# Attention scores in 64-row products, one head in each half of the array's rows

## The chip, the cores and the metric

The kernel runs on one core of a Trainium2 chip. A core has TensorE (matmuls; PE in the profile, and PEld for its weight loads), VectorE (DVE), ScalarE (ACT), GpSimd (POOL) and SyncE (SP), which here issues nearly all DMAs. The metric is the time of one execution on the device in microseconds, as the median of several runs.

## What is computed

Attention with 4 batches, 8 heads, 576 positions and 64 dimensions a head, in which each query keeps only its 32 largest scores, and behind it two feed-forward layers (512 to 2048 to 512) over the 2304 rows.

```python
scores = scale * np.matmul(q, k.transpose(0, 1, 3, 2))
kth = np.partition(scores, -32, axis=-1)[..., -32:-31]
scores = np.where(scores >= kth, scores, -1e9)
attn = softmax(scores)                      # over the keys
x = concat_heads(attn @ v)                  # 2304 x 512
h = x @ w_in;   x = g(h) @ w_out            # g: 0 below -1, h above 1, (h + 1)^2 / 4 between
h = np.maximum(x @ w_in2, 0); out = (h * h) @ w_out2
```

## The kernel before

**Precision.** Scores and the feed-forward products need more than one pass of the fast fp32r type. Each operand is split into a part "hi" (rounded to fp32r) and a rest "lo", and hi x hi, hi x lo and lo x hi are summed in PSUM.

**Slots.** Attention runs in 72 slots. A slot takes two units t = 0 and 1, each of 128 queries against all 576 keys. In slots 0 to 63 ("normal") the two units are the two heads of a pair, for the same 128 queries of one batch. In slots 64 to 71 ("packed") a unit holds the last 64 queries of both heads of a pair. Slots 0 to 3 ("raw") use unsplit fp32 inputs straight from kq0, with 64 dimensions on 64 rows of the array: head t lies on rows 64t to 64t + 63 (score_raw, L569, in two matmuls of 288 keys; fp32 makes two instructions of each).

**A slot on the engines.** Order is written out by hand in the slot() of each engine; engines meet only through semaphores.
- TensorE in slot n: scores of unit (n+1, 0), transposes of the probabilities of (n-1, 0) (turn_main, L623), scores of (n+1, 1), transposes of (n-1, 1) (L623, L629), then probabilities times v of slot n-1 (times_v, L645 and L650). Between these stand up to three steps of the feed-forward layers: up (L691, 12 matmuls) and down (L719 for the first layer, L725 for the second, 12 of 256 or 6 of 512 columns), placed by the table UP_POS, from slot 10 on.
- ScalarE copies the scores from PSUM into one of four tiles s_sb (copy_scores, L800), which it may do once the mask of the unit four earlier is done, and computes the exponentials (L821).
- VectorE finds the 32nd largest score with four MAX8 and three MATCH_REPLACE8 passes a unit (rank, L1054 and L1056), fourteen a slot. Its first pass over unit (n, t) waits for that unit's copy.
- POOL compares (L1232) and multiplies the mask in (L1237); turn_main waits for that.
- SP loads and stores. Of each pair of heads, keys and queries come once as kq_lo, are split into kq_hi and kq_lo and stored to kq_scratch (restack, L394, L395), and come back as ks (L399) and qs (L406) for each use.

**The score block before.** Rows of kq are interleaved by head (d, h), so that the reload in the form "(x d) h c" puts the hi part of one head on rows 0 to 63 and its lo part on rows 64 to 127, with the two heads side by side in the columns. One matmul over 128 rows thus gives hi x hi + lo x lo with variant 0 of the queries (hi over lo) and the two mixed products with variant 1 (lo over hi); kq_scratch has a third plane, a second copy of the hi queries, to make variant 1. A normal unit takes four matmuls of 288 keys (L588), a packed one ten (L598, L601, L603, L606), since both heads have to be summed into one tile.

score_ps has two PSUM banks, columns 0 to 287 and 512 to 799; the next unit's scores wait until ScalarE has copied them (s_copied).

## Time and profile before

| | us |
|---|---|
| median of 3 runs | 1234.5 (1234.43 to 1236.56) |
| profiled execution | 1234.88 |
| its span in the trace | 1233.1 |
| TensorE busy (matmuls) | 1178.1 |
| VectorE busy | 839.2 |
| ScalarE busy | 776.8 |
| POOL busy | 740.9 |

The span is what the trace covers; 1.8 us of the execution lie around it. Busy times are sums over the whole span, and the engines' shares change from stretch to stretch: up to about slot 10 there is attention alone, then attention and feed-forward steps together until 915 us, then feed-forward steps alone. The records give a matmul's length from its start to its modelled end, and the next one starts before that end; the distance between two starts is what a matmul costs in a dense row. A few matmul records are missing. "L588" is line 588 of the kernel before.

### The profile page before, as it was taken

What the parts mean: (1) busy time and instruction counts of PE and PEld (TensorE: products, weight loads), DVE (VectorE), ACT (ScalarE), POOL (GpSimd) and SP (SyncE); (2) the same over time, 40 slices, a digit from 0 to 9 for tenths busy, and PEclk for the clock granted to TensorE, in tenths of its full rate; (3) what the DMA queues carried; (4) which work ended last, traced back from release to release, by engine and by line L of the source; (5) the groups of instructions that cost most, each with busy time, mean ns of one, the idle gap of its engine ahead of it and who ended that gap; (6) DMA issues with size and microseconds to landing.
All of it is one profiled execution on the core that took longest, in us unless ns stands there. A gap on an engine that the chain in (4) does not pass through costs nothing.

```text
span 1233.1 us, 23032 instructions
## 1 busy us (share of the span) xinstructions
PE 1178.1 (96%) x8184; PEld 1092.9 (89%) x8184; DVE 839.2 (68%) x1863; ACT 776.8 (63%) x1672; POOL 740.9 (60%) x589
## 2 busy tenths in 40 slices
PE   6777899999999999999999999999999999999998
PEld 4667888998889999999999999999999888998887
DVE  7999999999987799899899987878740111110000
ACT  7877666786765767767776665666654544653343
POOL 6868786888977767777676766665652222222222
PEclk9967999999999999999999999999999999999999
DMA  6767886777869932334458831456339500780000
GB/s 253 278 242 262 283 320 259 267 244 308 331 225 396 383 113 99 136 111 138 138 189 296 299 116 40 141 189 191 126 131 368 194 1 1 313 336 1 1 35 18
DMA packets 94914, 239.45 MB, mean 194 GB/s; under 512 B 7760, under 2 KB 46672, under 8 KB 82512
## 3 DMA queue, kind: packets, MB, share of 16 engines
q1 hardware_dynamic: 94640, 237.71, 53.4%
q8 instruction: 66, 1.08, 0.3%
q14 instruction: 48, 0.39, 0.1%
q10 hardware_dynamic: 160, 0.26, 0.1%
HBM read 166.12 MB, written 71.83 MB: 193 GB/s over the span
## 4 chain that ended last, share of the span: by engine, by line
PE 74%; POOL 9%; ACT 7%; issue 4%; DVE 3%; DMA 2%; SPq 1%; ACTq 0%; POOLq 0%
PE h_ps L691 22%; PE y_ps L725 11%; PE y_ps L719 10%; PE pv_ps L650 6%; PE score_ps L691 6%; PE tr_ps L623 4%; PE score_ps L588 3%; POOL s_sb L1232 3%; POOL prob L1237 3%; POOL kq_lo L1215 2%; PE y_ps L711 2%; PE y_ps L714 2%; PE tr_ps L714 2%; PE tr_ps L711 2%; DVE top L1054 1%
## 5 line engine op out<-in xcount | busy, mean ns | idle before, releaser
L691 PE MATMUL h_ps<-xt_ks,w_in 128*128 128x256 f32 (+1 forms) x2628 | 384.8, 296 | 2.2 <-ACT rg L931 1.4
L691 PEld LDWEIGHTS h_ps<-xt_ks,w_in 128*128 128x128 f32 x2628 | 341.8, 191 | 12.3 <-ACT rg L931 1.9
L1250 POOL TENSOR_TENSOR g_lo<-rg,g_hi 128x256 fp32r<-128x256 f32 x224 | 169.4, 756 | 281.6 <-ACT g_hi L949 165.8
L1054 DVE MAX8 top<-rest 128x8 f32<-128x576 f32 x432 | 304.5, 746 | 0.4
L1232 POOL TENSOR_SCALAR s_sb<-s_sb,top 128x576 f32<-128x576 f32 x126 | 222.1, 1763 | 33.8 <-DVE top L1054 33.8
L1056 DVE MATCH_REPLACE8 rest<-top,rest 128x576 f32<-128x576 f32 x288 | 211.4, 741 | 0.0
L1237 POOL TENSOR_TENSOR prob<-s_sb,prob 128x576 f32<-128x576 f32 x128 | 183.0, 1432 | 14.9 <-ACT s_sb L842 3.1
L719 PE MATMUL y_ps<-g_hi,w_out 128*128 128x256 f32 x896 | 180.9, 285 | 4.9 <-POOL g_lo L1250 4.5
L725 PE MATMUL y_ps<-w_out,g_hi 128*128 128x512 f32 x448 | 158.6, 395 | 0.8 <-ACT moves L910 0.7
L719 PEld LDWEIGHTS y_ps<-g_hi,w_out 128*128 128x128 f32 x896 | 147.6, 192 | 7.0 <-POOL g_lo L1250 5.7
L650 PE MATMUL pv_ps<-v_sb,pt 128*128 128x65 f32 x1024 | 129.9, 283 | 0.0
L650 PEld LDWEIGHTS pv_ps<-v_sb,pt 128*128 128x128 f32 x1024 | 128.1, 204 | 0.0
L719 PE MATMUL y_ps<-g_lo,w_out 128*128 128x256 f32 x448 | 126.8, 283 | 0.0
L800 ACT ACTIVATE s_sb<-score_ps 128x576 f32<-128x576 f32 x143 | 91.9, 643 | 48.7 <-PE score_ps L588 27.2
L623 PE MATMUL tr_ps<-ident,prob 128*128 128x128 f32 x576 | 95.5, 292 | 17.8 <-POOL prob L1237 17.6
L1054 DVE MAX8 top<-s_sb 128x8 f32<-128x576 f32 x144 | 102.3, 743 | 14.9 <-ACT s_sb L800 14.8
L1117 DVE SCALAR_TENSOR_TENSOR rg<-rg 128x256 f32<-128x256 f32 x112 | 62.8, 561 | 63.7 <-ACT rg L942 63.4
L1056 DVE MATCH_REPLACE8 rest<-top,s_sb 128x576 f32<-128x576 f32 x144 | 105.6, 739 | 0.1
L821 ACT ACTIVATE prob<-s_sb,neg_max 128x576 f32<-128x576 f32 x128 | 99.4, 776 | 2.1
L725 PEld LDWEIGHTS y_ps<-w_out,g_hi 128*128 128x128 f32 x448 | 84.6, 189 | 17.4 <-issue 1.2
L588 PE MATMUL score_ps<-xt_ks,qs_g 128*128 128x288 f32 x480 | 91.0, 315 | 7.4 <-DMA qs_g<-kq_scratch 6.2
L623 PEld LDWEIGHTS tr_ps<-ident,prob 128*128 128x128 f32 x576 | 72.2, 149 | 27.1 <-issue 20.1
(122 smaller groups left out, 1819.9 us busy)
## 6 DMA issues: line engine op xcount, KB each, us to landing
w_in<-w_scratch SPq DMA_DIRECT2D x32, 1024.0 KB, 7.1
w_out<-w_scratch SPq DMA_DIRECT2D x32, 1024.0 KB, 8.2
xt_ks<-kq_scratch SPq DMA_DIRECT2D x46, 576.0 KB, 6.4
qs_g<-kq_scratch SPq DMA_DIRECT2D x152, 128.0 KB, 4.2
w_scratch<-w_in SPq DMA_DIRECT2D x16, 1024.0 KB, 7.3
w_scratch<-w_out SPq DMA_DIRECT2D x16, 1024.0 KB, 7.0
v_sb<-in_vv_dram SPq DMA_DIRECT2D x48, 325.0 KB, 6.4
moves<-in_w_dram SPq DMA_DIRECT2D x27, 512.0 KB, 6.5
```

Source lines behind the costliest of these rows:

```text
L588: last = pe.matmul(score_ps[:, 512 * half:512 * half + HALF], qq[:, t, var, :], kk[:, t, HALF * half:HALF * (half + 1)], start=(var == 0), ...
L623: last = pe.transpose(tr_ps[t][:, P * j:P * (j + 1)], prob[n % 2][:, base + P * j:base + P * (j + 1)], ident[:, :])
L650: last = pe.matmul(pv_ps[:, V1 * t:V1 * (t + 1)], pt[:, base + P * j:base + P * (j + 1)], vb[:, V1 * (2 * j + t):V1 * (2 * j + t + 1)], st ...
L691: last = pe.matmul(h_bank(k), wi[:, f // 2, w, m, cols], x_part(k, x, m), start=(m == 0 and n == 0), stop=(m == KT - 1 and n == 2))
L719: last = pe.matmul(y_ps[i][:, CHUNK * (m % 2):CHUNK * (m % 2 + 1)], wo[:, f // 2, w, f % 2, P * m:P * (m + 1)], g[f % 2][:, :], start=(f = ...
L725: last = pe.matmul(y_ps[i][:, :], g[f % 2][:, P * i:P * (i + 1)], wo[:, f // 2, w, f % 2, :], start=(f == 0 and n == 0), stop=(f == FT - 1 ...
L821: act.activation(pr[:, SEQ * t:SEQ * (t + 1)], s_sb[i][:, :], ACT.Exp, bias=bias[:, t:t + 1], scale=SCALE).then_inc(exp_done, 1)
L1054: dve.max(best, src[:, :]).then_inc(rank_step, 1)
L1056: dve.match_replace(rest[t][:, :], best, src[:, :], LOWEST).then_inc(rank_step, 1)
L1232: pool.tensor_scalar(s[:, :], s[:, :], top[n % 2][:, t, TOPK - 1:TOPK], None, ALU.is_ge).then_inc(keep_done, 1)
L1237: pool.tensor_tensor(pr[:, cols], s[:, :], pr[:, cols], ALU.mult).then_inc(masked, 1)
L1250: pool.tensor_tensor(lo_of(k), u_of(k), hi_of(k).bitcast(F32), ALU.subtract).then_inc(g_lo_done, 1)
```

## The change

**Layout.** Rows of kq are now head-major: head h on rows 64h to 64h + 63, hi and lo in two planes x of ks and qs. kq_scratch loses its third plane. A load of qs is one DMA, not two, and the third store of restack is gone. For packed slots a new load_tail_ks brings the keys in three DMAs, so that both heads' keys stand in the same order.

**Normal slots from 4 on.** Unit t no longer stands for head t in the score block, but for half t of the keys. Three products (hi x hi, hi x lo, lo x hi) are made for either head on its own 64 rows of the array, head h into bank h: six matmuls of 64 rows and 288 keys, with the head as inner loop. The copy of block t goes to half t of both heads' tiles, so that VectorE's first pass (rank) waits for both copies of the slot.

**Packed slots.** Six matmuls of 128 rows and 288 keys; the queries of the other head are zeros in the layout.

**Tiles.** Six score tiles in three pairs instead of four, and the copy waits for the masks of the slot three earlier. qs_g is half as large; the corner of the second packed unit moves to kq_lo, and the wide jobs' tiles for odd steps to g_all.

```diff
-    kq_dram = [scratch(f"kq_scratch{g}", [3, 2 * DIM, KQ]) for g in range(PREPS)]
+    kq_dram = [scratch(f"kq_scratch{g}", [2, P, KQ]) for g in range(PREPS)]
...
-        s_sb = [sb(f"s_sb{i}", [P, SEQ]) for i in range(4)]
+        s_pairs = sb("s_pairs", [P, 3, 2 * SEQ])
+        s_sb = [s_pairs[:, i // 2, SEQ * (i % 2):SEQ * (i % 2 + 1)] for i in range(6)]
...
+        def in_halves(n):
+
+            return RAW_SLOTS <= n < NORMAL
...
-                sp.dma_start(kq_dram[g][2, :, SEQ:KQ], kq_hi[:, SEQ:KQ].bitcast(F32)).then_inc(restacked, 16)
...
                 sp.dma_start(ks[i][:, :, :].bitcast(F32),
-                             kq_dram[g][0:2, :, 0:SEQ].rearrange("x (d h) c -> (x d) h c", h=2)
+                             kq_dram[g][:, :, 0:SEQ].rearrange("x p c -> p x c")
                              ).then_inc(ks_loaded[i], 16)
+
+            def load_tail_ks(g, i):
+                sp.wait_ge(restacked, 16 * 2 * (PREP_ORDER.index(g) + 1))
+                for rows, to, cols in ((slice(0, DIM), slice(0, SEQ), slice(0, SEQ)),
+                                       (slice(DIM, P), slice(0, MAIN), slice(TAIL, SEQ)),
+                                       (slice(DIM, P), slice(MAIN, SEQ), slice(0, TAIL))):
+                    sp.dma_start(ks[i][rows, :, to].bitcast(F32),
+                                 kq_dram[g][:, rows, cols].rearrange("x p c -> p x c")
+                                 ).then_inc(ks_loaded[i], 16)
 
             def load_qs(g, t, i):
                 cols = slice(SEQ + P * t, SEQ + P * (t + 1))
-                for var in range(2):
-                    sp.dma_start(qs[i][:, :, var, :].bitcast(F32),
-                                 kq_dram[g][var:var + 2, :, cols].rearrange("x (d h) n -> (x d) h n", h=2)
-                                 ).then_inc(qs_loaded[i], 16)
+                sp.dma_start(qs[i][:, :, :].bitcast(F32),
+                             kq_dram[g][:, :, cols].rearrange("x p n -> p x n")).then_inc(qs_loaded[i], 16)
...
-                    for var in range(2):
-                        for half in range(2):
-                            last = pe.matmul(score_ps[:, 512 * half:512 * half + HALF], qq[:, t, var, :],
-                                             kk[:, t, HALF * half:HALF * (half + 1)],
-                                             start=(var == 0), stop=(var == 1))
+                    for i, (x, y) in enumerate(products):
+                        for h in range(2):
+                            rows = slice(DIM * h, DIM * (h + 1))
+                            last = pe.matmul(score_ps[:, 512 * h:512 * h + HALF], qq[rows, x, :],
+                                             kk[rows, y, HALF * t:HALF * (t + 1)],
+                                             start=(i == 0), stop=(i == 2))
...
-                    for var in range(2):
+                    for i, (x, y) in enumerate(products):
                         for half in range(2):
-                            pe.matmul(score_ps[:, 512 * half:512 * half + HALF], qq[:, 0, var, :],
-                                      kk[:, 0, HALF * half:HALF * (half + 1)],
-                                      start=(var == 0), stop=False, skip_group_check=True)
...
+                            last = pe.matmul(score_ps[:, 512 * half:512 * half + HALF], qq[:, x, :],
+                                             kk[:, y, HALF * half:HALF * (half + 1)],
+                                             start=(i == 0), stop=(i == 2))
...
-                if u >= 4:
-                    act.wait_ge(masked, u - 3)
+                if n >= 3:
+                    act.wait_ge(masked, 2 * (n - 3) + 2)
...
+                if in_halves(n):
+                    pair = s_pairs[:, n % 3, :].rearrange("p (h k) -> p h k", h=2)
+                    act.activation(pair[:, :, HALF * t:HALF * (t + 1)], banks, ACT.Copy).then_inc(s_copied, 1)
+                    return
...
                 if op == 0:
-                    dve.wait_ge(s_copied, 2 * n + t + 1)
+                    dve.wait_ge(s_copied, 2 * n + (2 if in_halves(n) else t + 1))
...
-            rows, tail_rows = slice(hh, P, 2), slice(DIM * hh, DIM * (hh + 1))
+            rows = tail_rows = slice(DIM * hh, DIM * (hh + 1))
```

Below stands the built order of instructions at the places of which the prediction speaks. Rows read: line, operation, what it writes <- what it reads, size, how many in a row.

TensorE, a normal slot with first-layer steps, before: y_ps<-g_hi is the last down matmul, score_ps the score block, tr_ps the transposes, h_ps the next up step.

```order
L719 MATMUL y_ps<-g_lo,w_out 128x256
L719 MATMUL y_ps<-g_hi,w_out 128x256
L588 MATMUL score_ps<-xt_ks,qs_g 128x288 x4
L623 MATMUL tr_ps<-ident,prob 128x128 x4
L629 MATMUL tr_ps<-ident,prob 128x128
L691 MATMUL h_ps<-xt_ks,w_in 128x256 x12
```

The same place in the changed program:

```order
L737 MATMUL y_ps<-g_all,w_out 128x256 x12
L614 MATMUL score_ps<-xt_ks,qs_g 128x288 x6
L641 MATMUL tr_ps<-ident,prob 128x128 x4
L647 MATMUL tr_ps<-ident,prob 128x128
L709 MATMUL h_ps<-xt_ks,w_in 128x256 x12
```

The block stands where it stood, between down and the transposes, with six matmuls for four (the rows don't print that each reads 64 rows). The down steps are the same twelve; they read as one row since g_hi and g_lo are now one tensor.

TensorE, a packed slot with second-layer steps, before:

```order
L725 MATMUL y_ps<-w_out,g_hi 128x512
L598 MATMUL score_ps<-xt_ks,qs_g 128x288 x2
L601 MATMUL score_ps<-xt_ks,qs_g 128x288
L603 MATMUL score_ps<-xt_ks,qs_g 128x224
L606 MATMUL score_ps<-xt_ks,qs_g 128x64
L598 MATMUL score_ps<-xt_ks,qs_g 128x288 x2
L601 MATMUL score_ps<-xt_ks,qs_g 128x288
L603 MATMUL score_ps<-xt_ks,qs_g 128x224
L606 MATMUL score_ps<-xt_ks,qs_g 128x64
L623 MATMUL tr_ps<-ident,prob 128x128 x4
```

and in the changed program:

```order
L743 MATMUL y_ps<-w_out,g_all 128x512 x6
L624 MATMUL score_ps<-xt_ks,qs_g 128x288 x6
L641 MATMUL tr_ps<-ident,prob 128x128 x4
L709 MATMUL h_ps<-xt_ks,w_in 128x256 x12
L743 MATMUL y_ps<-w_out,g_all 128x512 x6
```

Ten matmuls with small ones among them have become six equal ones, at the same place.

## Rows read from the trace of the kernel before

**Rows 1.** The page, part 1: busy us (share of the span) xinstructions.

```profile
PE 1178.1 (96%) x8184; PEld 1092.9 (89%) x8184; DVE 839.2 (68%) x1863; ACT 776.8 (63%) x1672; POOL 740.9 (60%) x589
```

**Rows 2.** Busy time in stretches (from:to us), length, engines, granted clock, DMA share, GB/s.

```profile
core 0: us, PE busy (x) PEld busy (x) DVE busy (x) ACT busy (x) POOL busy (x), PEclk, DMA share, GB/s
40.00:200.00 160.00, 130.95 (x881) 121.45 (x881) 156.83 (x354) 116.80 (x225) 123.92 (x78) 0.87 0.76 277
200.00:788.00 588.00, 579.52 (x4567) 560.55 (x4565) 528.64 (x1166) 405.25 (x919) 434.15 (x334) 1.00 0.59 211
788.00:915.00 127.00, 126.74 (x924) 119.15 (x923) 94.02 (x228) 77.79 (x189) 80.62 (x79) 1.00 0.48 154
74.00:77.00 3.00, 2.92 (x12) 2.10 (x10) 3.00 (x9) 2.64 (x5) 3.00 (x3) 0.50 0.96 362
```

**Rows 3.** Score matmuls of normal blocks, 200 to 788 us: count, ns min/median/max, first and last.

```profile
L588 PE MATMUL score_ps<-xt_ks,qs_g x360: 291/295/401, 205.0 to 775.2; 128*128 128x288 f32 x180
```

**Rows 4.** Timeline, PE, a block at full clock: start us, length us (a row's whole), instruction.

```profile
570.13 0.28 PE L719 MATMUL y_ps<-g_hi,w_out 128*128 128x256 f32 x1
570.25 0.69 PE L588 MATMUL score_ps<-xt_ks,qs_g 128*128 128x288 f32 x4
570.78 0.60 PE L623 MATMUL tr_ps<-ident,prob 128*128 128x128 f32 x4
571.14 0.36 PE L691 MATMUL h_ps<-xt_ks,w_in 128*128 128x256 f32 x1
```

**Rows 5.** Timeline, PE, raw scores of slots 0 and 1.

```profile
4.66 0.85 PE L569 MATMUL y_ps<-pt 64*128 64x288 f32 x1
5.01 0.69 PE L569 MATMUL score_ps<-pt 64*128 64x288 f32 x1
5.30 0.68 PE L569 MATMUL y_ps<-pt 64*128 64x288 f32 x1
5.49 0.68 PE L569 MATMUL score_ps<-pt 64*128 64x288 f32 x1
...
7.75 2.29 PE L569 MATMUL score_ps<-pt 64*128 64x288 f32 x4 [0.80 <-ACT s_sb L796]
```

**Rows 6.** Timeline, PE, edges of blocks: into 64 rows, out, and without change of rows.

```profile
22.02 0.42 PE L623 MATMUL tr_ps<-ident,prob 128*128 128x128 f32 x1
22.37 0.84 PE L569 MATMUL score_ps<-rg 64*128 64x288 f32 x1
...
23.97 0.69 PE L569 MATMUL score_ps<-rg 64*128 64x288 f32 x1
24.58 0.69 PE L623 MATMUL tr_ps<-ident,prob 128*128 128x128 f32 x2
...
75.47 0.44 PE L588 MATMUL score_ps<-xt_ks,qs_g 128*128 128x288 f32 x1
75.71 0.41 PE L623 MATMUL tr_ps<-ident,prob 128*128 128x128 f32 x1
```

**Rows 7.** Timeline, PEld (weight loads), the load behind the transposes.

```profile
571.11 0.19 PEld L691 LDWEIGHTS h_ps<-xt_ks,w_in 128*128 128x128 f32 x1
```

**Rows 8.** Waits of PE from 200 to 790 us, the longest: us in total, times, longest.

```profile
PE tr_ps L623 <- POOL prob L1237: 4.1, 7, 1.1
```

**Rows 9.** Timeline, PE, a packed block: its first matmuls and the transposes behind it.

```profile
826.40 0.42 PE L598 MATMUL score_ps<-xt_ks,qs_g 128*128 128x288 f32 x2
...
827.56 0.66 PE L623 MATMUL tr_ps<-ident,prob 128*128 128x128 f32 x4
```

**Rows 10.** Timeline, DVE and ACT, start of slot 6; in brackets idle time and what ended it.

```profile
66.56 0.74 DVE L1054 MAX8 top<-s_sb 128x8 f32<-128x576 f32 x1
67.82 0.76 DVE L1054 MAX8 top<-s_sb 128x8 f32<-128x576 f32 x1 [0.52 <-ACT s_sb L800]
...
67.15 0.64 ACT L800 ACTIVATE s_sb<-score_ps 128x576 f32<-128x576 f32 x1
```

**Rows 11.** DMA issues: out<-in engine xcount, KB each, us to landing.

```profile
qs_g<-kq_scratch SPq DMA_DIRECT2D x152, 128.0 KB, 4.2
...
kq_scratch<-kq_hi SPq DMA_DIRECT2D x16, 320.0 KB, 4.7
```

More of the change, by code:

```diff
@@ L224, in build @@
         neg_max = [sb(f"neg_max{i}", [P, 2]) for i in range(2)]
-        prob = [sb(f"prob{i}", [P, 2 * (MAIN + P)]) for i in range(2)]
+        prob = [sb(f"prob{i}", [P, 2 * SEQ]) for i in range(2)]
         pt = sb("pt", [P, 2 * (MAIN + P)])
@@ L231, in build @@
         g_sb = [rg[:, 2 + i, :] for i in range(2)]
-        g_hi = [sb(f"g_hi{i}", [P, CHUNK], F32R) for i in range(2)]
-        g_lo = [sb(f"g_lo{i}", [P, CHUNK], F32R) for i in range(2)]
+        g_all = sb("g_all", [P, 4 * CHUNK], F32R)
+        g_hi = [g_all[:, 2 * CHUNK * i:2 * CHUNK * i + CHUNK] for i in range(2)]
+        g_lo = [g_all[:, 2 * CHUNK * i + CHUNK:2 * CHUNK * (i + 1)] for i in range(2)]
         ident = sb("ident", [P, P])
@@ L358, in lo_of, with s_of, corner @@
         def lo_of(k):
-            return (kq_hi, qs_g)[k % 2][:, 2 * CHUNK:4 * CHUNK] if wide(k // FT) else g_lo[k % 2][:, :]
+            if not wide(k // FT):
+                return g_lo[k % 2][:, :]
+            return kq_hi[:, 2 * CHUNK:4 * CHUNK] if k % 2 == 0 else g_all[:, 2 * CHUNK:4 * CHUNK]
+        def s_of(u):
+            return s_sb[u % 6]
+        def corner(n, t):
+            if t == 0:
+                return prob[n % 2][:, MAIN:MAIN + P]
+            return kq_lo[:, P * (n % 2):P * (n % 2 + 1)].bitcast(F32)
+        def in_halves(n):
+            return RAW_SLOTS <= n < NORMAL
         def raw(p):
@@ L579, in score @@
                     return
-                if not packed(n):
-                    if n % 2 == 0:
-                        pe.wait_ge(ks_loaded[(n // 2) % 2], 16 * (n // 4))
+                products = ((0, 0), (0, 1), (1, 0))
+                if in_halves(n):
                     if t == 0:
-                        pe.wait_ge(qs_loaded[n % 2], 16 * 2 * (n // 2 - 1))
+                        if n % 2 == 0:
+                            pe.wait_ge(ks_loaded[(n // 2) % 2], 16 * (n // 4))
+                        pe.wait_ge(qs_loaded[n % 2], 16 * (n // 2 - 1))
@@ L597, in score @@
                         for half in range(2):
-                            pe.matmul(score_ps[:, 512 * half:512 * half + HALF], qq[:, 0, var, :],
-                                      kk[:, 0, HALF * half:HALF * (half + 1)],
-                                      start=(var == 0), stop=False, skip_group_check=True)
-                        pe.matmul(score_ps[:, 0:HALF], qq[:, 1, var, :], kk[:, 1, TAIL:TAIL + HALF],
-                                  start=False, stop=(var == 1), skip_group_check=True)
@@ L603, in score @@
-                        pe.matmul(score_ps[:, 512:512 + MAIN - HALF], qq[:, 1, var, :],
-                                  kk[:, 1, TAIL + HALF:SEQ],
-                                  start=False, stop=(var == 1), skip_group_check=True)
-                        last = pe.matmul(score_ps[:, 512 + MAIN - HALF:512 + HALF], qq[:, 1, var, :],
-                                         kk[:, 1, 0:TAIL],
-                                         start=False, stop=(var == 1), skip_group_check=True)
+                            last = pe.matmul(score_ps[:, 512 * half:512 * half + HALF], qq[:, x, :],
+                                             kk[:, y, HALF * half:HALF * (half + 1)],
+                                             start=(i == 0), stop=(i == 2))
@@ L630, in turn_shared @@
                 if packed(n):
-                    last = pe.transpose(tr_ps[0][:, P:2 * P], prob[n % 2][:, 2 * MAIN + P:2 * MAIN + 2 * P],
+                    last = pe.transpose(tr_ps[0][:, P:2 * P], corner(n, 1),
                                         ident[:, :])
@@ L795, in copy_scores @@
                     for half in range(2):
-                        last = act.activation(s_sb[1][:, HALF * half:HALF * (half + 1)], y_ps[half][:, 0:HALF],
+                        last = act.activation(s_of(1)[:, HALF * half:HALF * (half + 1)], y_ps[half][:, 0:HALF],
                                               ACT.Copy)
@@ L811, in exponentiate @@
             def exponentiate(n, t):
-                i = (2 * n + t) % 4
+                s = s_of(2 * n + t)
                 if t == 0:
@@ L824, in exponentiate @@
                     base = (MAIN + P) * t
-                    act.activation(pr[:, base:base + MAIN], s_sb[i][:, 0:MAIN], ACT.Exp,
+                    act.activation(pr[:, base:base + MAIN], s[:, 0:MAIN], ACT.Exp,
                                    bias=bias[:, t:t + 1], scale=SCALE)
                     for hh in range(2):
-                        rows, col = slice(TAIL * hh, TAIL * (hh + 1)), base + MAIN + TAIL * hh
-                        last = act.activation(pr[rows, col:col + TAIL], s_sb[i][rows, MAIN:SEQ], ACT.Exp,
+                        rows = slice(TAIL * hh, TAIL * (hh + 1))
+                        last = act.activation(corner(n, t)[rows, rows], s[rows, MAIN:SEQ], ACT.Exp,
                                               bias=bias[rows, t:t + 1], scale=SCALE)
@@ L1318, in lay_out @@
             vv[:, p, tail_rows, at + DIM] = 1.0
-    for hh in range(2):
-        kq0[:, DIM * hh:DIM * (hh + 1)] = kq[0, 0:RAW_SLOTS // 2, hh::2, 0:RAW]
+    kq0[:] = kq[0, 0:RAW_SLOTS // 2, :, 0:RAW]
     blocks = []
```

41 lines of the change are left out of this document (21 added, 20 removed).

## The prediction, made before the changed kernel ran

> **What bounds the kernel now.** The page's first part comes first: TensorE is busy 96% of the span, VectorE 68% [rows 1]. Those are averages, so the span is next cut into stretches by what limits them [rows 2]. From 40 to 200 us VectorE is busy 156.8 of 160 us (the 14 rank passes of each slot) and TensorE only 131: here only what delays VectorE costs time, and TensorE has 29 us to spare. From 200 to 788 us TensorE is busy 579.5 of 588 us and VectorE 528.6. "Busy" flatters TensorE, whose ends are modelled, so I checked it by distances between starts: around 570 us matmul follows matmul without a hole, 0.12 us apart at 256 columns and 0.13 at 288 [rows 4], and in the whole stretch TensorE's longest wait in sum is the one of L623 for POOL's mask, 4.1 us [rows 8]. So from 200 us on, whatever is put on TensorE's queue is paid in full. 788 to 915 us (packed slots) is the same, 126.7 of 127. Behind it no scores are made. The granted clock is 1.00 (2.4 GHz) from 200 us on, 0.87 on average before.
>
> So the change is to be counted on TensorE: 90 score blocks lie in the bound stretch (360 recorded matmuls of L588, four to a block [rows 3]), 28 more lie ahead of it, and 16 packed blocks lie behind.
>
> **Part 1, the normal score block: six 64-row matmuls for four 128-row ones.** The block now: last matmul of down() starts at 570.13, the four scores at 570.25, the transposes behind them at 570.78 [rows 4]. That is 0.12 + 0.53 = 0.65 us from the last down matmul to the first transpose, nothing lost at either edge.
>
> Do the two halves of the array work side by side? The trace has one place that tells, the first slot, where the raw scores of both heads stand in the queue together: rows 0 to 63 write score_ps, rows 64 to 127 y_ps. score_ps starts at 5.01 and 5.49, y_ps between them at 5.30 [rows 5] and again at 5.78, so each half steps by 0.48 us. Where one half works alone, four such matmuls take 2.29 us with 0.69 for the last, again about 0.5 a step [rows 5, 6]. The halves do not slow each other. So six matmuls should take three steps of 0.13 us instead of four: **-0.13 us a block**.
>
> What do the edges cost? The same raw blocks stand between 128-row transposes. No granted clock is recorded there, but a transpose is 0.42 long as at 75 us [rows 6], where the granted clock is 0.50, that is 1.2 GHz [rows 2]. The last 64-row matmul starts at 23.97 and is 0.69 long; its own step is 0.48, yet the transpose behind it starts only at 24.58, 0.61 later, about 0.07 before the modelled end of the 64-row one [rows 6]. Two more such edges, at 32.8 and 36.1 us, are 0.61 too. The other way, the transpose from 22.02 is 0.42 long and the 64-row matmul starts at 22.37, again 0.07 before the end, 0.35 after it where the transposes' own step is 0.21 [rows 6]. The counter-example is the 128-row block at 75 us: the last L588 starts at 75.47, is 0.44 long, and the transpose behind it starts at 75.71, 0.24 later [rows 6], the plain step of 288 columns at that clock, with 0.2 of the earlier one still to run. So TensorE empties itself whenever the number of rows changes, and nothing else in these places differs in the same manner: rows decide, not the kind of matmul. The Trainium skill says this as a rule (TensorEngine Tiling (Array Packing), Key Properties: changing the tiling mode drains the engine); it gives no duration, and by that rule the trace agrees.
>
> The drain also takes away that the next weights are loaded ahead. At full clock a weight load that was not ahead starts at 571.11 [rows 7], and the matmul it serves starts at 571.14 but is 0.36 long instead of 0.28 [rows 4]: its stream starts 0.11 after the load.
>
> Worked out at full clock, from those rows (an estimate, since no row shows a change of rows at 2.4 GHz):
> - into the block: 0.28 - 0.07 = 0.21 instead of 0.12, and 0.11 for the load: +0.20 us
> - out of it: 0.30 - 0.07 = 0.23 instead of 0.13, and 0.05 for the transposes' load (at half clock 24.58 + 0.69 - 0.42 = 24.85, so 0.27 to the second one instead of 0.21 [rows 6]): +0.15 us
> - three steps for four: -0.13 us
>
> That is **+0.21 us a block**, and 90 x 0.21 = **+19 us**. Both ends: without any edge cost -0.13 (-12 us); with loads in turn (below) +0.48 (+43 us).
>
> The 28 blocks before 200 us cost TensorE as much or more, some 7 us, in its 29 us of slack: nothing, as long as the copy behind them isn't late for VectorE (part 3).
>
> **Part 2, the packed block: six 128-row matmuls for ten.** Now 826.40 to 827.56, 1.16 us [rows 9]; six of 288 columns are 6 x 0.13 = 0.79. No change of rows here. 16 x 0.37 = **-6 us**, all on the bound engine. The keys come in three DMAs instead of one, issued a slot ahead of their use and behind nothing new, so the two more issues stay hidden.
>
> **Part 3, both heads from one pair of copies.** VectorE's first pass over a unit now waits for the second copy, not for the first. In most slots that copy is 2 to 5 us ahead. In slot 6 it isn't: the first pass starts at 66.56, the second copy runs from 67.15 to 67.79, and the second pass already waits 0.52 [rows 10]. The first pass would start at 67.82 too: 0.74 us more. Slots 4 and 8 are like it, together at most 1.9 us in the stretch that VectorE bounds. In nine or so slots after 365 us the copy is late as well, but there VectorE has slack; at worst some of the 0.74 comes back as TensorE waiting for a mask, 5 us at most. Against it: with three pairs of score tiles the copy waits for a mask one slot older. TensorE's waits for POOL are the 4.1 us of [rows 8], and longer slots give VectorE and POOL more room, so down to -4. I take **+1.5**, near the early slots, which have rows.
>
> **Part 4, DMA and SP.** 76 of 152 loads of qs and the 16 third stores of 320 KB go [rows 11]: 15 MB less, and 92 issues fewer on SP (less 32 more for the packed keys). TensorE waits for none of them after 200 us, so 0; below, -1 from the early slots. The wide jobs' tiles have only moved: 0.
>
> **Sum.** +19 - 6 + 1.5 = +14.5 us on the profiled execution's 1234.9 (span 1233.1 and 1.8 around it), that is 1249.4; the median of the runs lies 0.4 lower: **1249**. Its own range by the bounds is 1242 to 1258.
>
> **Rivals.**
> *The loads of the two halves go in turn.* A load takes the 0.11 of [rows 7], and the rows at the start of the program are too wide apart to show whether two loads run together. If they queue, six loads are 0.66 us and become the step: 0.27 more a block, 90 x 0.48 - 6 + 1.5 = +39, **1274**. For it: loads are the densest thing the engine does. Against it: the halves behaved as independent in all else. The Trainium skill states that a load's time depends on columns, not rows (TensorE: Matmul & The Clock Gate, LDWEIGHTS), so that twelve loads a slot would cost half as much again as eight; it also has loads overlap where row groups differ (Part 3 of the same page). No run here shows which.
>
> *A gain: no drain in the dense stream.* If the edge cost seen at half clock came from an empty queue and is hidden when the queue is full, each block saves its 0.13: -12 - 6 = -18, **1217**. It decides if the edge costs under 0.13 a block. Against it: three edges agree within 0.01 us, and the semaphores of the two later ones had long been reached. The Trainium skill's table of theoretical speed-up (TensorEngine Tiling, Overview), twice for contractions up to 64, gives this sign.
>
> *Half the edge cost.* If the loads do go ahead and only the emptying is paid, 0.09 + 0.09 - 0.13 = 0.05 a block: +4.5 - 6 + 1.5 = 0, **1235**, no change.
>
> *VectorE becomes the bound* through the later first pass: 12 slots at 0.74 on top of the forecast, up to **1258 to 1266**.
>
> **How the numbers follow.** Forecast 0.52, loads in turn 0.18, gain 0.12, half the edge 0.10, VectorE 0.08. The range of 1234 to 1276 holds all but the gain and a part of the half-edge case. A measurement here can tell 0.2%, 2.5 us, from no change: faster 0.13, same 0.08, slower 0.79.
>
> **What would show it.** On the timeline around a normal block after 200 us: about 0.32 us from the last down matmul to the streaming of the first score, pairs of starts 0.13 apart, and 0.28 to the transposes; the mean length of a slot 0.4 us up; 788 to 915 shorter by 6 us; the part behind it unchanged in length. Pairs 0.21 apart mean the loads go in turn. Starts without a hole at the edges mean I was wrong about the drain, and the time falls.

## The result and the profile after

The changed kernel takes **1242.6 us** (median of 5 runs, 1242.14 to 1244.64); the kernel before, on the same chip, 1234.9 (5 runs). The ratio is 1.0062 with a 95% interval of 1.0052 to 1.0073: **0.6% slower**. The forecast was 1249.0 with a range of 1234 to 1276. The sign and the mechanism held, but its sum was 14.5 us and only 8.4 came in the span. The profiled execution of the changed kernel took 1243.26 us, its span is 1241.5, against 1233.1 before. Of one kernel below, m_four_edges, the profiled execution ran at a granted clock of about 0.55 from 118 us on and took 1971 us, so its time is that of its three other runs.

Part 1 of the page and the stretches of [rows 2], now of the changed kernel (busy us, share of the span or number of instructions in brackets; in the second view then the granted clock, the DMA share and GB/s):

```profile
PE 1197.5 (96%) x8360; PEld 1077.0 (87%) x8360; DVE 841.8 (68%) x1863; ACT 777.8 (63%) x1672; POOL 742.8 (60%) x589
...
40.00:200.00 160.00, 142.00 (x950) 125.11 (x950) 157.61 (x357) 117.67 (x226) 124.42 (x79) 0.86 0.71 256
200.00:788.00 588.00, 582.91 (x4655) 537.23 (x4655) 520.08 (x1142) 399.07 (x904) 427.05 (x327) 1.00 0.53 191
788.00:915.00 127.00, 123.85 (x886) 115.80 (x886) 101.74 (x242) 80.48 (x196) 82.67 (x80) 1.00 0.57 141
```

The bound is where it was. From 40 to 200 us TensorE has 11 us more to do and takes them from its slack: VectorE is busy 157.6 of 160 us, 156.8 in [rows 2]. From 200 us on TensorE is busy 583 of 588 us. The number that stands out is in the third stretch: TensorE was busy 126.74 of 127 us there [rows 2] and is now busy 123.85.

A normal block at full clock answers to [rows 4]. Timeline, PE and then PEld, changed kernel (start us, length us, instruction). The view joins neighbours into one row; rows cut narrower are shown between:

```profile
567.31 0.28 PE L737 MATMUL y_ps<-g_all,w_out 128*128 128x256 f32 x1
567.52 0.40 PE L614 MATMUL score_ps<-xt_ks,qs_g 64*128 64x288 f32 x2
567.52 0.53 PE L614 MATMUL score_ps<-xt_ks,qs_g 64*128 64x288 f32 x4
567.52 0.66 PE L614 MATMUL score_ps<-xt_ks,qs_g 64*128 64x288 f32 x6
567.89 0.29 PE L614 MATMUL score_ps<-xt_ks,qs_g 64*128 64x288 f32 x2
568.12 0.66 PE L641 MATMUL tr_ps<-ident,prob 128*128 128x128 f32 x4
...
567.52 0.19 PEld L614 LDWEIGHTS score_ps<-xt_ks,qs_g 64*128 64x128 f32 x2
567.52 0.30 PEld L614 LDWEIGHTS score_ps<-xt_ks,qs_g 64*128 64x128 f32 x4
```

- In: 567.31 to 567.52, 0.21 us instead of 0.12, and the first pair is 0.40 long instead of 0.29, since its load, at 567.52 too, was not ahead.
- Inside: two matmuls start together, and each further pair ends 0.13 later (0.40, 0.53, 0.66). The loads behave alike: two take 0.19, four 0.30. Both halves load and stream side by side (in the records two matmuls of a pair start 3 to 4 ns apart).
- Out: the last pair starts at 567.89, the transposes at 568.12, 0.23 later. Four of them are 0.66 long instead of 0.60, the load again.

Over the 76 blocks between 240 and 780 us with a down step ahead, the median from its last matmul to the first transpose is 0.822 us, against 0.656 before, and the transposes behind take 0.057 more: 0.88 against 0.66, **+0.22 us a block**. The forecast had +0.21.

The score matmuls in the stretch of [rows 3], and TensorE's waits there, against [rows 8] (us in total, times, longest):

```profile
L614 PE MATMUL score_ps<-xt_ks,qs_g x540: 286/292/405, 204.4 to 787.0; 64*128 64x288 f32 x180
...
PE tr_ps L641 <- POOL prob L1259: 3.1, 8, 0.9
```

**Where the 8.4 us are.** The score blocks of slots 4 to 71 stand on TensorE in the same order in both kernels, so each block's start can be compared. They are numbered from 4 (slot 4, unit 0) to 139 (slot 71, unit 1). Differences of the starts, after less before:

| block | before us | after us | difference |
|---|---|---|---|
| 16 | 100.84 | 100.46 | -0.4 |
| 38 | 230.14 | 229.64 | -0.5 |
| 124, the first packed one | 783.54 | 795.49 | +11.9 |
| 139, the last | 888.39 | 897.15 | +8.8 |

So up to 230 us the new blocks cost nothing. Of the 86 distances from block to block behind it, 59 grew by 0.19 to 0.25 us, together 12.9; the other 27 sum to -0.4. In 18 of these 27 a wait of TensorE for POOL, ScalarE or another engine stands in the trace of the kernel before. Two more (43 and 45) grew by 0.5 and 1.1, with new waits of some 0.3 us in the changed kernel, and seven grew by 0.05 to 0.13 with no wait on record in either. What the 18 are shows at one of them. Timeline, PE, before and after, with the wait in brackets:

```profile
595.59 0.69 PE L588 MATMUL score_ps<-xt_ks,qs_g 128*128 128x288 f32 x4
596.65 0.63 PE L623 MATMUL tr_ps<-ident,prob 128*128 128x128 f32 x4 [0.37 <-POOL prob L1237]
```

```profile
602.91 0.68 PE L614 MATMUL score_ps<-xt_ks,qs_g 64*128 64x288 f32 x6
603.76 0.63 PE L641 MATMUL tr_ps<-ident,prob 128*128 128x128 f32 x4 [0.16 <-POOL prob L1259]
```

Block to transposes took 1.06 us before, though a block that waits for nothing takes 0.53 [rows 4]: TensorE stood still for 0.53 us, of which the row shows 0.37, since the matmul ahead has a modelled end. After, the transposes again start when POOL's mask is there, 0.85 us on, and the longer block has only filled the hole.

**The packed slots.** Timeline, PE, changed kernel, the block that answers to [rows 9], and block 134, some 30 us later:

```profile
835.79 0.95 PE L624 MATMUL score_ps<-xt_ks,qs_g 128*128 128x288 f32 x6
836.58 0.60 PE L641 MATMUL tr_ps<-ident,prob 128*128 128x128 f32 x4
...
866.32 1.03 PE L624 MATMUL score_ps<-xt_ks,qs_g 128*128 128x288 f32 x6 [2.30 <-DMA qs_g<-kq_scratch]
```

A block is 0.79 long as forecast, and its transposes are 0.60 long where [rows 9] had 0.66: they no longer stand behind a 64-column matmul. Each distance shrank by 0.43 (from the last block to the end it is 0.38), 16 x 0.43 = -6.9 us. One alone, into block 134 (the scores of slot 69, whose loads SP issues in its slot 67; the expectations call the place slot 67), grew by 2.8: it holds the wait of 2.30, and without it would have shrunk as well, so it costs 3.2. That wait was not there before. Some 0.6 of the other 0.9 are two waits for ScalarE in the same distance, a new one of 0.16 (the h_ps row) and one of 0.69 where before it was 0.26 (the y_ps rows); they stand in the other kernels with six-matmul packed blocks too (a, c, g, i, k and l). Waits of TensorE from 788 to 915 us, changed kernel and then before (us in total, times, longest):

```profile
PE y_ps L743 <- ACT moves L932: 0.7, 1, 0.7
PE h_ps L709 <- ACT rg L953: 0.2, 1, 0.2
...
PE y_ps L725 <- ACT moves L910: 0.3, 1, 0.3
```

SP's queue ahead of it, changed kernel and then kernel before (start us, length us, line, out<-in):

```profile
847.47 0.36 SPq L519 DMA_DIRECT2D moves<-y_scratch  x1
857.79 0.34 SPq L506 DMA_DIRECT2D out_dram<-moves  x1
858.22 1.92 SPq L425 DMA_DIRECT2D xt_ks<-kq_scratch  x3
860.19 0.60 SPq L431 DMA_DIRECT2D qs_g<-kq_scratch  x1
```

```profile
849.24 0.34 SPq L482 DMA_DIRECT2D out_dram<-moves  x1
849.68 0.53 SPq L399 DMA_DIRECT2D xt_ks<-kq_scratch  x1
850.26 1.39 SPq L406 DMA_DIRECT2D qs_g<-kq_scratch  x2
```

In both kernels SP has nothing issued for about 10 us ahead of the store of a finished output tile (from 847.47 to 857.79 here), and the loads of keys and queries stand behind it. Before, the store went 6.2 us ahead of the score block that needs them (855.41), and the loads were just in time. Now three key DMAs of 1.92 us stand ahead of the queries, and the queries take longer to land: 5.8 us in the median of the stretch from 855 to 870, against 4.4 from 848 to 858 in the kernel before. Why is not shown: a store of 512 KB stands ahead of them in both. (DMA issues: KB each, us from issue to landing, changed kernel.)

```profile
out_dram<-moves SPq DMA_DIRECT2D x1, 512.0 KB, 3.6
qs_g<-kq_scratch SPq DMA_DIRECT2D x3, 128.0 KB, 5.8
```

Together: -0.5 + 12.4 - 6.9 + 3.2 = +8.2 us, and +8.4 in the span.

### The profile page after: what moved, and what is told of

Same layout as the page of the kernel before. It is cut to its first block, busy times and chain, and to the rows that moved or that the text cites. A ratio compares the mean times of both kernels' runs of the same rounds, so it can differ in the third digit from the quotient of the medians.

```text
span 1241.5 us, 23292 instructions
## 1 busy us (share of the span) xinstructions
PE 1197.5 (96%) x8360; PEld 1077.0 (87%) x8360; DVE 841.8 (68%) x1863; ACT 777.8 (63%) x1672; POOL 742.8 (60%) x589
## 4 chain that ended last, share of the span: by engine, by line
PE 78%; POOL 7%; DVE 5%; ACT 4%; issue 2%; DMA 2%; SPq 0%; ACTq 0%; POOLq 0%
PE h_ps L709 23%; PE y_ps L743 11%; PE y_ps L737 10%; PE pv_ps L668 7%; PE score_ps L709 6%; PE tr_ps L641 5%; PE score_ps L614 4%; DVE top L1076 3%; POOL s_pairs L1254 2%; DVE rest L1078 2%; POOL prob L1259 2%; PE y_ps L729 2%; PE y_ps L732 2%; PE tr_ps L729 2%; PE tr_ps L732 2%
## 5 line engine op out<-in xcount | busy, mean ns | idle before, releaser
L1272 POOL TENSOR_TENSOR g_all<-rg,g_all 128x256 fp32r<-128x256 f32 x224 | 170.0, 759 | 292.9 <-ACT g_all L971 162.5
L1254 POOL TENSOR_SCALAR s_pairs<-s_pairs,top 128x576 f32<-128x576 f32 x126 | 223.5, 1774 | 31.2 <-DVE top L1076 31.2
L1259 POOL TENSOR_TENSOR prob<-s_pairs,prob 128x576 f32<-128x576 f32 x128 | 182.6, 1429 | 16.0 <-DVE top L1076 4.5
L737 PE MATMUL y_ps<-g_all,w_out 128*128 128x256 f32 x1344 | 180.7, 284 | 3.1 <-POOL g_all L1272 3.1
L743 PE MATMUL y_ps<-w_out,g_all 128*128 128x512 f32 x672 | 174.1, 394 | 0.7 <-ACT moves L932 0.7
L737 PEld LDWEIGHTS y_ps<-g_all,w_out 128*128 128x128 f32 x1344 | 169.1, 191 | 5.2 <-POOL g_all L1272 4.3
L743 PEld LDWEIGHTS y_ps<-w_out,g_all 128*128 128x128 f32 x672 | 119.1, 189 | 21.5 <-issue 0.9
L1076 DVE MAX8 top<-s_pairs 128x8 f32<-128x576 f32 x144 | 101.8, 742 | 19.1 <-ACT s_pairs L823 10.0
L1078 DVE MATCH_REPLACE8 rest<-top,s_pairs 128x576 f32<-128x576 f32 x144 | 105.5, 738 | 0.1
L843 ACT ACTIVATE prob<-s_pairs,neg_max 128x576 f32<-128x576 f32 x128 | 99.2, 775 | 2.1
```

What stands on the lines that cost most here:

```text
L737: last = pe.matmul(y_ps[i][:, CHUNK * (m % 2):CHUNK * (m % 2 + 1)], wo[:, f // 2, w, f % 2, P * m:P * (m + 1)], g[f % 2][:, :], start=(f = ...
L743: last = pe.matmul(y_ps[i][:, :], g[f % 2][:, P * i:P * (i + 1)], wo[:, f // 2, w, f % 2, :], start=(f == 0 and n == 0), stop=(f == FT - 1 ...
L843: act.activation(pr[:, SEQ * t:SEQ * (t + 1)], s[:, :], ACT.Exp, bias=bias[:, t:t + 1], scale=SCALE).then_inc(exp_done, 1)
L1076: dve.max(best, src[:, :]).then_inc(rank_step, 1)
L1078: dve.match_replace(rest[t][:, :], best, src[:, :], LOWEST).then_inc(rank_step, 1)
L1254: pool.tensor_scalar(s[:, :], s[:, :], top[n % 2][:, t, TOPK - 1:TOPK], None, ALU.is_ge).then_inc(keep_done, 1)
```

## The experiments

Twelve kernels ran. Each ratio is against the kernel before as timed beside that kernel. "Block" below is the median from the last matmul ahead to the first transpose, as above.

### What a block is made of: a to d

**a_four128** makes four matmuls of 128 rows in the changed kernel's layout and order.

```diff
-                    for i, (x, y) in enumerate(products):
+                    for i, (x, y) in enumerate(products[0:2]):
                         for h in range(2):
-                            rows = slice(DIM * h, DIM * (h + 1))
+                            rows = slice(0, P)
...
-                                             start=(i == 0), stop=(i == 2))
+                                             start=(i == 0), stop=(i == 1))
```

> The changed kernel, but a normal score block is four 128-row matmuls of 288 keys (two of the three products, over all 128 rows, so the scores of both heads are summed and the lo x hi product is left out). Everything else of the change stays: copies in halves, three pairs of tiles, fewer DMAs, six-matmul packed blocks. If changing the number of rows is what costs: 0.12 us into the block, four steps of 0.13, 0.13 out of it, 0.65 us in all instead of 0.86, the 59 or so blocks that pay give back 0.21 each, about 1230 us, and faster than the kernel before by what the packed blocks bring. If the later first pass of VectorE or the copies are what costs: no less than 1240.

**b_six128** has the line of rows alone changed: all six matmuls on 128 rows.

```diff
-                            rows = slice(DIM * h, DIM * (h + 1))
+                            rows = slice(0, P)
```

> The changed kernel, but each of the six matmuls of a normal block reads all 128 rows (the scores of both heads are summed). No change of rows at the edges, and no two matmuls side by side. Drain theory: 0.12 + 5 x 0.13 + 0.14, 0.91 us a block against 0.86, so 59 x 0.05 = +3 us, about 1246. If the edges cost nothing and the six matmuls themselves are the price: the same 1242 to 1243 with the same block. If two halves side by side were worth nothing: the block would be shorter than in the changed kernel, below 1240.

**c_four64** has the first and the last line of a's diff: four matmuls of 64 rows.

> The changed kernel with four 64-row matmuls a block (the lo x hi product is left out). Drain theory: one step of 0.13 less, both edges unchanged at 0.21 and 0.22: 0.73 us a block, about 59 x 0.13 = 8 us less, 1235. It differs from four 128-row matmuls by the edges less two steps, 0.08 a block. If the price lies in the matmuls (loads in turn): 0.21 less a block or more, 1230 or less.

| | us | ratio, 95% interval | in | block | between transposes | block 38 to 124 |
|---|---|---|---|---|---|---|
| before | 1234.5 | 1 | 0.120 | 0.656 | 0.108 | 0 |
| changed kernel | 1242.6 | 1.0062 (1.0052 to 1.0073) | 0.209 | 0.822 | 0.165 | +12.4 |
| a_four128 | 1229.4 | 0.9958 (0.9944 to 0.9972) | 0.120 | 0.653 | 0.109 | -0.9 |
| b_six128 | 1248.2 | 1.0111 (1.0096 to 1.0126) | 0.120 | 0.918 | 0.108 | +17.7 |
| c_four64 | 1233.1 | 0.9988 (0.9979 to 0.9998) | 0.209 | 0.674 | 0.165 | +4.3 |

Blocks of a, b and c in the timeline (start us, length us):

```profile
572.74 0.69 PE L614 MATMUL score_ps<-xt_ks,qs_g 128*128 128x288 f32 x4
573.26 0.60 PE L641 MATMUL tr_ps<-ident,prob 128*128 128x128 f32 x4
```

```profile
571.45 0.96 PE L614 MATMUL score_ps<-xt_ks,qs_g 128*128 128x288 f32 x6
572.25 0.60 PE L641 MATMUL tr_ps<-ident,prob 128*128 128x128 f32 x4
```

```profile
572.70 0.53 PE L614 MATMUL score_ps<-xt_ks,qs_g 64*128 64x288 f32 x4
573.16 0.66 PE L641 MATMUL tr_ps<-ident,prob 128*128 128x128 f32 x4
```

The edges, and nothing else, follow the rows: 0.209 in and 0.165 between the first transposes wherever the block has 64 rows, 0.120 and 0.11 wherever it has 128. Nothing else differs between a and c, or between b and the changed kernel: the number type, which at the edges of [rows 6] differed too (raw fp32 scores), is the same here. Their price comes out twice, with equal numbers of matmuls. c against a: 0.674 + 0.057 - 0.653 = +0.08 although two steps of 0.13 are saved (two steps are 0.265, b less a), so 0.34 us. The changed kernel against b: 0.88 - 0.92 = -0.04 with three steps saved, 0.36 us. Both halves at once are a real gain of 0.13 a pair, and a change of rows and back costs some 0.35.

The blocks came as expected (0.65, 0.91 and 0.73 with the transposes), the times within 2.2 us: 1229.4 for 1230, 1248.2 for 1246, 1233.1 for 1235. Run b also answers to the count of 59: its block is 0.26 longer than before, 62 of the 86 distances grew by 0.24 to 0.29, 16.3 us, and the other 24 by 1.4 together. All 24 are among the 27 above: the places that do not pay lie in the program, not in the 64 rows. That b is 5.3 us above the changed kernel in these distances, 0.06 each where a block says 0.04, is not accounted for.

Run a also bounds all the rest of the change: everything but the 64-row matmuls stands in it, and it is faster than the kernel before by 0.4%.

**d_head_outer** takes the order of the six matmuls: first all three of head 0, then all three of head 1.

```diff
-                    for i, (x, y) in enumerate(products):
-                        for h in range(2):
+                    for h in range(2):
+                        for i, (x, y) in enumerate(products):
```

> The changed kernel with the head as outer loop: three matmuls on rows 0 to 63, then three on rows 64 to 127, the same six. If each half of the rows has a queue of its own and takes its matmuls as they come, the second three start beside the first: 0.86 us a block and 1242.6. If matmuls start in the order of the program, they come one after another: 0.21 + 0.11 + 5 x 0.13 + 0.28 = 1.25 us a block, 0.39 more, up to 59 x 0.39 = 23 us: 1265.

It took 1243.4 us, 1.0073 (1.0058 to 1.0088), the changed kernel's time. Timeline, PE:

```profile
563.19 0.40 PE L614 MATMUL score_ps<-xt_ks,qs_g 64*128 64x288 f32 x1
563.19 0.41 PE L614 MATMUL score_ps<-xt_ks,qs_g 64*128 64x288 f32 x2
563.19 0.56 PE L614 MATMUL score_ps<-xt_ks,qs_g 64*128 64x288 f32 x4
563.19 0.69 PE L614 MATMUL score_ps<-xt_ks,qs_g 64*128 64x288 f32 x6
```

The second matmul to start does so 10 ns after the first. In program order the first three read the same 64 rows and would be 0.13 apart, so the one that starts beside the first is the fourth: each half takes its own matmuls from the queue. The rows don't name the half, so this is concluded from the starts. The Trainium skill says otherwise (TensorE: Matmul & The Clock Gate, Part 3: Packing small matmuls), that matmuls start and end in program order; this trace does not agree, and the order of the two heads is worth nothing (the block's median is 0.828 for 0.822).

### The copies and the pairs of score tiles: e and j

**e_both_copies** is the kernel before, with VectorE's first pass waiting for both copies.

```diff
-                    dve.wait_ge(s_copied, 2 * n + t + 1)
+                    dve.wait_ge(s_copied, 2 * n + (2 if RAW_SLOTS <= n < NORMAL else t + 1))
```

> The kernel before with one wait changed: VectorE's first pass over a unit of a normal slot waits for both copies of the slot. The forecast's part 3 gave this 0 to 1.9 us in the early slots and up to 5 behind them: 1235 to 1240. If the first pass is never what is late, because the slots of before that have a late second copy are few: 1234.5 to 1236.5, with slots 4, 6 and 8 longer by up to 0.7 each.

1235.2 us in ten runs, 0.9999 (0.9990 to 1.0009). Block 4 starts 0.65 us late, block 16 on time, block 38 0.6 late, and by block 124 nothing of it is left (-0.1). The wait costs nothing that ten runs can tell.

**j_two_pairs** is the changed kernel with two pairs of score tiles (the four tiles' room that the kernel before had) instead of three.

```diff
-        s_pairs = sb("s_pairs", [P, 3, 2 * SEQ])
+        s_pairs = sb("s_pairs", [P, 2, 2 * SEQ])
...
-                if n >= 3:
-                    act.wait_ge(masked, 2 * (n - 3) + 2)
+                if n >= 2:
+                    act.wait_ge(masked, 2 * (n - 2) + 2)
...
-                    pair = s_pairs[:, n % 3, :].rearrange("p (h k) -> p h k", h=2)
+                    pair = s_pairs[:, n % 2, :].rearrange("p (h k) -> p h k", h=2)
```

> The changed kernel with two pairs of score tiles instead of three, so that ScalarE's copy for slot n waits for both masks of slot n - 2. If the third pair is what keeps the halves from costing VectorE time: in the early stretch the copy waits for the second mask of the slot just before, a few us each slot, and VectorE starts each slot late, 10 slots and more by 1 to 3 us: 1255 to 1275. If it is idle there: 1242 to 1244.

1339.0 us, 1.0841 (1.0826 to 1.0856), 96 more than the changed kernel. Waits (us in total, times, longest), and the stretch from 200 us, of j:

```profile
ACT s_pairs L821 <- POOL prob L1259: 146.7, 59, 5.9
...
200.00:788.00 588.00, 527.57 (x4129) 480.69 (x4130) 451.90 (x1002) 349.62 (x800) 379.69 (x289) 0.99 0.51 183
```

In the changed kernel the copy waits for the scores and hardly for a mask:

```profile
ACT s_pairs L821 <- PE score_ps L614: 29.9, 46, 2.3
ACT s_pairs L821 <- POOL prob L1259: 2.8, 4, 1.1
```

A block fills half of both heads' tiles, so its copy needs both masks of a slot, and with two pairs those of the slot that POOL is just at: 2.5 us in each of 59 waits, and TensorE idle for 60 of 588 us behind it. Both expectations were too low. The third pair is what the halves need to keep their pace; whether it would gain anything in the kernel before was not run.

### The packed slots and SP's queue: g, h, i, k and l

**g_packed_only** is the kernel before with the packed part alone: six matmuls on 128 rows, and keys reloaded by three DMAs.

```diff
-                    for var in range(2):
+                    for i, (x, y) in enumerate(((0, 0), (0, 1), (1, 0))):
...
+                            last = pe.matmul(score_ps[:, 512 * half:512 * half + HALF], qq[:, x, :],
+                                             kk[:, y, HALF * half:HALF * (half + 1)],
+                                             start=(i == 0), stop=(i == 2))
```

> The kernel before with the packed blocks alone changed: head-major rows for the packed keys and queries only (three loads of keys and two of queries), six 128-row matmuls for ten. 16 blocks at 0.43 us less as measured in the changed kernel, 6.9 us, less what late loads cost in slot 67 (2.7 us in the changed kernel; here one load more): 1229 to 1231.

1231.5 us (1228.35 to 1233.05), 0.9963 (0.9949 to 0.9978). Each packed distance shrank by 0.43 again; the one into block 134 grew by 0.77, and TensorE waits there for the queries for 0.3 us. The six runs lie far apart, and the profiled one, at 1228.35, is the fastest; what the others lose has no trace.

Four more kernels move the packed slots' loads on SP. **h_packed_early** is g and **i_after_early** the changed kernel, with the loads issued ahead of position 3n + 2 of SP's slot n instead of behind it (a slot has three positions, 3n to 3n + 2, at which stores and loads of the feed-forward layers stand):

```diff
+                if n > NORMAL and n - NORMAL + 2 in range(SLOTS - NORMAL):
+                    for t in range(2):
+                        load_packed(2 * (n - NORMAL + 2) + t)
...
-                if n - NORMAL + 2 in range(SLOTS - NORMAL):
+                if n <= NORMAL and n - NORMAL + 2 in range(SLOTS - NORMAL):
```

> The same, and SP issues a packed slot's loads ahead of the store that it stood behind in slot 67. If the stall of 2.7 us there is SP waiting for that store and issuing the key loads behind it, it goes: 1227 to 1228. If it is the DMAs' own time: as without the move, 1229 to 1231.

> The changed kernel with the packed slots' loads issued ahead of that store. SP theory: TensorE's wait of 2.3 us for qs in slot 67 is gone, 1239.9 instead of 1242.6. If the loads themselves are slow: 1242 to 1243.

h took 1228.8 us, 0.9947 (0.9934 to 0.9959), i 1242.9, 1.0063 (1.0051 to 1.0075). For i this was a miss, and my edit was the reason: store and y load stand at position 202, which is 3 x 67 + 1, still ahead of the new place. TensorE's wait for the queries only fell from 2.3 to 1.2 us. The same holds for h: SP's queue around the store is in h as in g, the distance into block 134 grew by 0.87 (0.77 in g) and the wait for the queries is 0.4 us. So h is no test of the place, its profiled execution of 1228.59 us is level with g's, and that its median lies 2.7 below g's is unexplained.

**k_after_ahead** and **l_packed_ahead** (the changed kernel, and g) have the same lines ahead of position 3n, and so ahead of store and y load.

> The changed kernel with the packed slots' loads issued before the y load and the store of slot 67 (the earlier move had left both of them ahead, as its trace shows). If that place in SP's order makes the stall: TensorE's wait for qs in slot 67 (2.3 us in the profile of the changed kernel, 1.2 in that of the earlier move) is gone, the packed blocks all 0.43 us shorter, 1240 to 1241.5. If it stays: about 1242.6.

> The kernel before with six-matmul packed blocks and the loads at the same earlier place: 16 x 0.43 = 6.9 us less than before without a stall, 1227.5 to 1228; with the stall of the runs of that kind 1228.8.

SP's queue in k:

```profile
850.85 1.89 SPq L425 DMA_DIRECT2D xt_ks<-kq_scratch  x3
852.78 0.60 SPq L431 DMA_DIRECT2D qs_g<-kq_scratch  x1
...
857.84 0.33 SPq L519 DMA_DIRECT2D moves<-y_scratch  x1
858.49 0.35 SPq L506 DMA_DIRECT2D out_dram<-moves  x1
```

k took **1240.8 us** (1240.52 to 1241.46), 1.0047 (1.0035 to 1.0060). The distance into block 134 grew by 0.3 instead of 2.8, TensorE waits for no DMA in the packed slots, and the span is +6.5 us against +8.4. So what made TensorE wait for the queries in the changed kernel was the place in SP's queue: 2.5 us less in this distance, 1.9 in the median. The size is less sure than the cause, for with the place unchanged the growth into block 134 is not the same from kernel to kernel: 2.8 in the changed one, 3.0 in d, 1.7 in b and i, 1.6 in a and 0.9 in c. l took 1228.8, 0.9956 (0.9942 to 0.9969). Its distance grew by 0.3 where g's grew by 0.8 and h's by 0.9, and no gain over h shows in the time.

h and l, at 1228.8 us and 0.4 to 0.5% below the kernel before, are **faster than both kernels**: the packed part of the change without its normal part.

### More changes of rows: m

**m_four_edges** puts the middle product of each block on 128 rows, so that a block has four changes of rows instead of two, and one step more.

```diff
-                            rows = slice(DIM * h, DIM * (h + 1))
+                            rows = slice(0, P) if i == 1 else slice(DIM * h, DIM * (h + 1))
```

> The changed kernel with the middle product of each normal block on all 128 rows (it sums both heads): the same six matmuls, but four changes of rows a block instead of two. Drain theory: two edges more, each 0.33 to the next start instead of 0.13 (0.40 or 0.36 long, less 0.07), less one pair that no longer runs side by side: 1.29 us from the last down matmul to the transposes instead of 0.82, so 0.47 a block on the 59 blocks that pay, or more, 1270. If only the first change of a block costs: 0.95 us a block, 1250.

1294.2 us, 1.0473 (1.0457 to 1.0489): 52 us above the changed kernel. One block in its trace (timeline, PE; the transposes behind it step by 0.21, the step of half clock [rows 6], the first by 0.27):

```profile
42.93 0.61 PE L614 MATMUL score_ps<-xt_ks,qs_g 64*128 64x288 f32 x2
42.93 1.14 PE L614 MATMUL score_ps<-xt_ks,qs_g 64*128 64x288 f32 x3
43.87 0.98 PE L614 MATMUL score_ps<-xt_ks,qs_g 128*128 128x288 f32 x3
44.24 0.61 PE L614 MATMUL score_ps<-xt_ks,qs_g 64*128 64x288 f32 x2
44.78 0.47 PE L641 MATMUL tr_ps<-ident,prob 128*128 128x128 f32 x1
```

From the first pair to the first matmul of 128 rows it is 0.53 us, from the last of them to the next pair 0.37, and out to the transposes 0.54, where the plain step of 288 columns is 0.24 [rows 6]. Changes inside a block cost like those at its edges: 0.53 and 0.54 out of 64 rows (the late load of the pair ahead is in both), 0.37 inside and 0.35 at an edge [rows 6] into them. The direction is right, the size was not: 28 us were expected. If every one of the 86 distances paid, 0.6 us each are needed. That a block longer by so much fills all the holes in which the changed kernel's blocks still hid is likely, but no trace at full clock shows it; it stays open.

## Why the prediction was right, and where its sum was off

- **What bounds the kernel.** Right from 230 us, not from 200: block 38 at 230 us still stands where it stood, and blocks 16 to 38 did not move (-0.1 us). What takes up the four longer blocks between 200 and 230 us is not shown: VectorE is busy 27.05 of these 30 us and TensorE 29.59. (Ahead of 200 us lie 30 blocks, 480 matmuls of L588 less the 360 of [rows 3], and not 28; no term hung on it.)
- **The halves side by side.** Right, pairs 0.13 apart. The rows of raw scores [rows 5] were enough to tell this; that loads run side by side as well they could not tell.
- **The edges.** Right in each piece: 0.21 in, 0.23 out, a load's 0.11 at the first pair and 0.05 to 0.06 at the transposes. The guess at full clock from rows at half clock came within 0.01 us a block (0.22 measured; the forecast's own terms, 0.20 + 0.15 - 0.13, give 0.22 too, which it wrote as 0.21). The distance to the transposes, forecast as 0.28 with the load in it, is 0.23 and 0.06.
- **90 x 0.21 = +19 us.** This term was mis-sized: it is 12.4. The price was right and the count wrong: 59 blocks paid. Four of the 31 that did not lie before 230 us; of the other 27, 18 are places where TensorE already waited for a mask or another engine, two had new waits, and seven grew by less with no wait on record. The step that failed is "whatever is put on TensorE's queue is paid in full", which took [rows 8], 4.1 us in 7 waits, for all there is; TensorE's waits of all kinds in that window come to 8.1 us in 16, and fell to 4.9 in 14. Rows with a wait understate it by what is modelled at the end of the matmul ahead (0.37 shown, 0.53 real, above), and by the same 0.16 a shorter wait would have no row at all, which is an estimate from this one place.
- **The packed block.** -6 forecast, -6.9 measured: 0.79 us a block was right, and the transposes behind it gave 0.05 more.
- **"The two more issues stay hidden."** Wrong. They were costed against "issued a slot ahead of their use", which was a slot ahead in program order; on SP's queue a store that waits stands ahead of them. 3.2 us in one place, of which 2.3 were TensorE waiting for the queries; a better place brought back 1.9 in the median (k). This stall is also why the total came as near as it did: without it the change would have cost some 5 us of the 14.5 forecast. That part of the hit is luck.
- **Both copies, +1.5.** Nothing: run e has 0.9999. In run e slot 6, on which the term rested [rows 10], has its wait of 0.56 us, now ahead of the first pass, and no time follows; in the changed kernel it has none. The first pass of unit 0 follows the pass ahead without idle time (timeline, DVE):

```profile
66.39 1.41 DVE L1076 MAX8 top<-rest 128x8 f32<-128x576 f32 x2
67.72 0.74 DVE L1076 MAX8 top<-s_pairs 128x8 f32<-128x576 f32 x1
```

  The change shifts the early slots among themselves: block 4 starts 0.75 us late and block 16 0.4 early.
- **DMA, 0.** The qs loads are 76 for 152 [rows 11], the traffic 15 MB less, and no time followed.
- **The rivals.** Loads in turn (1274) is refuted by loads that start together. No drain (1217) and half the edge cost (1235) are refuted by runs a to c: edges cost 0.34 to 0.36 us, where the step that they must pay for is 0.13. VectorE as bound did not come. The time lies midway between half the edge cost (1235) and the forecast (1249), but not through cheaper edges: a third of the blocks didn't pay, and the queries came late.

## What to carry to other kernels

Splitting the array by rows pays only for a long run of narrow matmuls: count the changes of rows, some 0.35 us for in and out at full clock, against what each pair saves, 0.13 us at 288 columns, and remember that hi and lo stacked on 128 rows had filled the array already. Where an engine is "busy 99%", compare distances between starts of the same work in loose and dense places to find the holes that modelled ends hide, for a longer step falls into them first. And cost a DMA by what waits ahead of it on its queue, not by how many slots ahead the program names it.

## What the runs showed of the hardware

- The two halves of 64 rows take matmuls and loads each for itself: the fourth in program order starts 10 ns after the first (run d), and two loads end within the 0.19 us of one.
- A change of the number of rows costs the same whichever way the work around it is arranged: at full clock 0.21 us to the next start into 64 rows (step before it 0.12), 0.23 out of them (0.13), and 0.11 and 0.06 us for loads that did not go ahead; at half clock, where the plain step is 0.24, 0.37 into 64 rows inside a block (run m), and 0.53 and 0.54 out of a pair whose own load was late.
- The transposes behind a matmul of 64 columns take longer: four transposes are 0.66 long behind it [rows 9] and 0.60 behind one of 288.
- Loads of 128 KB issued behind a store of 512 KB landed in 6.0 and 5.6 us in the changed kernel and in 4.3 to 4.7 in the kernel before; the same load issued ahead of the store landed in 3.5 to 4.0 (run k).
